# One reduction over 1152 columns instead of three partial ones: the row maximum of an attention score tile

## The chip, the cores and the metric

The program runs on one core of one Trainium2 chip. The metric is the device time of one execution in microseconds (us), of which the median of several runs is taken. A core has five engines that run their own instruction streams in order and meet at semaphores: TensorE (PE in the profile; its weight loads are PEld), VectorE (DVE), ScalarE (ACT), GpSimd (POOL) and SyncE (SP), which here issues the DMAs.

## The reference

Attention with queries pooled in pairs, then a soft mixture of experts, then a gated projection. The change is in the attention stage alone:

```python
def _attn_ref(q, k, v):          # 4 batches, 8 heads, 1152 positions, 64 wide
    q_pool = q.reshape(B, H, S // 2, 2, D).mean(axis=3)
    scores = scale * np.matmul(q_pool, k.transpose(0, 1, 3, 2))
    scores = scores - np.max(scores, axis=-1, keepdims=True)
    attn = np.exp(scores)
    attn = attn / (np.sum(attn, axis=-1, keepdims=True) + 1e-09)
    return np.matmul(attn, v)
...
x = moe(attn_out)                # 32 slots, 8 experts
g = x @ w_in - np.tanh(x @ w_in)
return g @ w_out
```

The kernel takes the row maximum over all 1152 keys before the exponential, as the reference does.

## The kernel before, in words

The attention stage goes over 16 pairs of heads. `over_pairs` writes out pairs 0, 1, 14 and 15 and puts pairs 2 to 13 into a loop of six passes with two pairs each; inside the loop the values that semaphores are waited for are computed in registers. A pair has twelve steps in a fixed order (`SEQ`): nine steps work on a tile of scores (T 0 to T 8: 128 queries by 1152 keys), and three prepare the next pair (Q at step 3, K at steps 6 and 9).

The scores of a tile lie in three banks of PSUM, 512, 512 and 128 columns (`CHUNK`), next to each other. Two such groups of banks ("slots") take turns, so the tile of step s reuses the slot of step s - 2. Around one tile the engines do this:

- TensorE in step s writes the three chunks of scores of step s's tile (`scores`, L304, two matmuls a chunk). Ahead of them it transposes chunks 0 and 1 of the probabilities of the tile of step s - 2 (`prob_chunk`, L320, eight transposes); this waits until the exponential of that tile is done (`exp_done`, L312). Between score chunks 1 and 2 it transposes the last block of that tile (L320, one transpose), which waits for VectorE's copy of chunk 1 (`second_evac`, L317). At the end of most steps come matmuls of transposed probabilities with V (`pv`, L337); steps 1, 3, 6 and 10 have none.
- VectorE in step s first copies chunk 1 of the transposed probabilities from PSUM to SBUF (L415, or L413 for the tile that mixes two heads; 512 columns). In steps 5 and 11 it then scales results (L447 to L461). After that it takes the partial maxima of score chunks 0 and 1, copies the last block of 128 transposed columns (`third`, L415), takes the partial maximum of chunk 2, and combines the three (L500) into one column of `neg_max`.
- ScalarE in step s copies chunk 0 of the transposed probabilities (L553) and then computes the exponential of the tile of step s - 1 over its 1152 columns (L542), which needs that tile's `neg_max` (`neg_done`). The exponential is followed by a read of its accumulator, the row sums.

Steps 5, 8 and 11 have no tile two steps back (a Q or K step lies there), so VectorE has no copies in them and TensorE no transposes of probabilities.

GpSimd prepares q and k of the next pair, SyncE loads k, q and v. Behind the attention stage follow the gating, the experts and the projection (`mlp`), which the change does not touch.

The tile step on VectorE is short enough to see here; L496 and L500 are the instructions that the change replaces:

Of the kernel before, what the change touches and what calls it, by code (L numbers as in the profile page):

```python
# [7 lines left out]
ALU = mybir.AluOpType  # L8
ACT = mybir.ActivationFunctionType
AX = mybir.AxisListType  # L10
P = 128
# [6 lines left out]
def attention(nc, dram, sizes, x, ident, rep, rep_ready, rep_step, early):  # L18
# [8 lines left out]
    CHUNK = [(0, 4), (4, 8), (8, 9)]  # L27
    NCH = len(CHUNK)
# [30 lines left out]
    with ExitStack() as ctx:  # L59
        def sb(name, shape, dt=F32):  # L60
            return ctx.enter_context(nc.sbuf_tensor(name, shape, dt))

        def sem(name):
            return ctx.enter_context(nc.semaphore(name))
# [15 lines left out]
        ones = sb("ones", [P, 1])  # L80
        ident_r = sb("ident_r", [P, P], F32R)
        outT = [sb(f"outT{g}", [P, GN[g]]) for g in range(2)]
        part_neg = sb("part_neg", [P, NCH])
        neg_max = sb("neg_max", [P, TILES])
        row_sum = [sb(f"row_sum{i}", [P, QT + 1, 2]) for i in range(2)]
        mix_sum = [sb(f"mix_sum{i}", [P, 1]) for i in range(2)]
# [6 lines left out]
        v_in = [sem("v_in0"), sem("v_in1")]  # L93
        zeroed, ident_ready = sem("zeroed"), sem("ident_ready")
        k_hi, k_split, q_sum = sem("k_hi"), sem("k_split"), sem("q_sum")
        part_done = sem("part_done")
        scores_full, neg_done, exp_done = sem("scores_full"), sem("neg_done"), sem("exp_done")
        ktr_full, k_evac, qtr_full, q_evac, q_high, q_low = (
            sem("ktr_full"), sem("k_evac"), sem("qtr_full"), sem("q_evac"), sem("q_high"), sem("q_low"))
# [11 lines left out]
        def wait(eng, s, value):  # L111

            if not isinstance(value, int) or value > 0:
                eng.wait_ge(s, value)
# [39 lines left out]
        def steps_of(last):  # L154
            return range(STEPS + DRAIN if last else STEPS)
# [83 lines left out]
        def slot_banks(s):  # L239
            return ps[:, 3 * (s % 2):3 * (s % 2) + 3, :]  # L240

        def slot_row(s):
            return slot_banks(s).rearrange("p b c -> p (b c)")[:, 0:S]
# [173 lines left out]
        def group_read(eng, p, j):  # L417

            if j == 0:
                wait(eng, pv_done, p * 2 - 1)  # L420
            elif j == G0:
                wait(eng, pv_done, p * 2)
# [8 lines left out]
        @block.vector  # L431
        def _(dve):
            dve.wait_ge(zeroed, 5)
            split(dve, 0)
            split_q(dve, 0, 0)

            def results(p, par, s, first):

                for g in range(2):
                    for b in (0, 1):  # L440
                        if OUT_STEP[g] == s + STEPS * b and not (b and first):
                            pp, q = p - b, par ^ b
                            if g == 0:

                                dve.wait_ge(exp_done, pp * TILES + TILES)
                                dve.wait_ge(mix_in, pp * 32 + 32)
                                nc.vector.tensor_scalar(row_den[:], row_sum[q][:], 1e-9, None, ALU.add).then_inc(den_done, 1)  # L447
                                dve.wait_ge(den_done, pp + 1)
                                nc.vector.reciprocal(row_inv[:], row_den[:]).then_inc(inv_done, 1)
                                dve.wait_ge(inv_done, pp + 1)  # L450
                            dve.wait_ge(otr_full, pp * 2 + g + 1)
                            n = 2
                            src = ps[:, TBANK, 0:n * P].rearrange("p (t h d) -> p t h d", t=n, h=2)
                            inv = row_inv[:, 2 * g:2 * g + n, :].unsqueeze(3).broadcast_to([P, n, 2, D])
                            dst = x[:, bass.ds(pp, 1), 2 * g:2 * g + n, :].rearrange("p o t (h d) -> p (o t) h d", h=2)
                            ins = nc.vector.tensor_tensor(dst, src, inv, ALU.mult)
                            if GN[g] > 2 * P:
                                src = ps[0:QR, TBANK, n * P:(n + 1) * P].rearrange("p (h d) -> p h d", h=2)
                                inv = row_inv[0:QR, QT, :].unsqueeze(2).broadcast_to([QR, 2, D])
                                dst = x[0:QR, bass.ds(pp, 1), QT, :].rearrange("p o (h d) -> p (o h) d", h=2)  # L460
                                ins = nc.vector.tensor_tensor(dst, src, inv, ALU.mult)  # L461
                            ins.then_inc(out_evac, 1)

            def body(p, par, first, last):
                for s in steps_of(last):
                    t2 = job_at(s, 2, first, last)
                    if t2 and t2[0] == "T":
                        _, j2, back = t2
                        pp = p - back
                        group_read(dve, pp, j2)  # L470
                        dve.wait_ge(ptr_full, (pp * TILES + j2) * NCH + 2)
                        evac_chunk(nc.vector.tensor_copy, s, j2, 1).then_inc(second_evac, 1)
                    results(p, par, s, first)

                    def third():

                        if t2 and t2[0] == "T":
                            dve.wait_ge(ptr_full, (pp * TILES + j2) * NCH + 3)
                            if job and job[0] == "T":
                                dve.wait_ge(scores_full, (p * TILES + job[1]) * NCH + 3)  # L480
                            elif job and job[0] == "K":
                                dve.wait_ge(ktr_full, (p + 1) * 2 + job[1] + 1)
                            elif job:
                                dve.wait_ge(qtr_full, p + 2)
                            evac_chunk(nc.vector.tensor_copy, s, j2, 2).then_inc(third_evac, 1)

                    job = job_at(s, 0, first, last)
                    if job and job[0] == "T":
                        tau = p * TILES + job[1]
                        j = job[1]  # L490
                        wait(dve, neg_done, tau)
                        for c in range(NCH):
                            if c == 2:
                                third()
                            dve.wait_ge(scores_full, tau * NCH + c + 1)
                            nc.vector.reduce_max(part_neg[:, c:c + 1], slot_banks(s)[:, c, 0:(CHUNK[c][1] - CHUNK[c][0]) * P], AX.X,  # L496
                                                 negate=True).then_inc(part_done, 1)
                        dve.wait_ge(part_done, tau * NCH + NCH)
                        wait(dve, exp_done, tau - TILES + 1)
                        nc.vector.tensor_scalar(neg_max[:, j:j + 1], part_neg[:, 0:1], part_neg[:, 1:2], part_neg[:, 2:3],  # L500
                                                ALU.min, ALU.min).then_inc(neg_done, 1)
                    else:
                        third()

            over_pairs(dve, body)

        @block.scalar
# [726 lines left out]
```

## Time and profile before

| | us |
|---|---|
| Median of 3 runs | 989.16 (988.77 to 993.28) |
| Profiled execution, its own time | 988.49 |
| Span of that execution in the trace | 986.7 |
| TensorE matmuls busy | 891.1 |
| VectorE busy | 597.8 |
| ScalarE busy | 497.0 |

The profile is of one execution. Its span leaves out 1.8 us that lie around the program. An engine's busy time is the sum over its instructions, over stages with different limits; where one engine waits for another is read from the idle time before an instruction and from what released it.

### The profile page before, as it was taken

To read this page: it belongs to the slowest core of one execution; us is meant where nothing else is said; L and a number is where in the kernel's file an instruction comes from. 1 tells how busy PE (TensorE), PEld (TensorE's weight loads), DVE (VectorE), ACT (ScalarE), POOL (GpSimd) and SP (SyncE) were. 2 spreads that over 40 slices of the span, in tenths; PEclk is the share of its full clock that TensorE was granted. 3 is DMA by queue.
4 is the path that set the end of the run, shared out by engine and by line. 5 is a ranking of instruction groups with operands and counts; after the bars stand their busy time and mean duration, and the time that the engine had idled before them with its cause. 6 is when DMAs were issued, how large, how long until landed. Compare 5 with 4: busy or idle time off the path is not lost. (4 is left out here: it accounts for less than half of the span.)

```text
span 986.7 us, 16399 instructions
## 1 busy us (share of the span) xinstructions
PE 891.1 (90%) x5707; PEld 644.4 (65%) x5707; DVE 597.8 (61%) x1175; ACT 497.0 (50%) x711; POOL 294.5 (30%) x207
## 2 busy tenths in 40 slices
PE   3999999999999999999999998876672899999998
PEld 2776776776776776776776765633231788888887
DVE  4676677677677677677677664420017866676770
ACT  1655555555555555555555553210016766666660
POOL 4353333333433333433433200000001343333441
PEclk9999999999999999999999999979885899999999
DMA  3312202202202202202202000949933100000000
GB/s 120 131 31 74 72 2 72 72 0 72 72 0 72 72 0 72 72 0 72 72 0 72 25 1 2 350 171 395 400 134 128 54 22 21 21 21 21 21 21 33
DMA packets 48865, 75.50 MB, mean 77 GB/s; under 512 B 5056, under 2 KB 23488, under 8 KB 48320
## 3 DMA queue, kind: packets, MB, share of 16 engines
q1 hardware_dynamic: 48832, 75.06, 22.3%
q8 instruction: 21, 0.34, 0.1%
q14 instruction: 12, 0.10, 0.0%
HBM read 70.32 MB, written 4.72 MB: 76 GB/s over the span
## 5 line engine op out<-in xcount | busy, mean ns | idle before, releaser
L496 DVE TENSOR_REDUCE part_neg<-ps 128x1 f32<-128x512 f32 (+1 forms) x432 | 220.8, 548 | 6.9 <-PE ps L304 6.6
L320 PE MATMUL ps<-ident,prob 128*128 128x128 f32 x1296 | 204.7, 285 | 19.1 <-DVE probT L415 9.2
L320 PEld LDWEIGHTS ps<-ident,prob 128*128 128x128 f32 x1296 | 143.2, 140 | 105.9 <-DVE probT L415 38.6
L415 DVE COPY probT<-ps 128x512 f32<-128x512 f32 (+1 forms) x256 | 125.1, 489 | 143.2 <-PE ps L320 116.8
L542 ACT ACTIVATE prob<-ps,neg_max 128x1152 f32<-128x1152 f32 x144 | 175.5, 1219 | 58.7 <-DVE neg_max L500 58.3
L304 PE MATMUL ps<-kT,qT_hi 128*128 128x512 f32 (+1 forms) x480 | 175.9, 383 | 5.3 <-DVE qT_lo L205 5.2
L553 ACT ACTIVATE probT<-ps 128x512 f32<-128x512 f32 x144 | 86.0, 597 | 171.6 <-PE ps L320 169.8
L337 PE MATMUL ps<-probT,v_nat 128*64 128x256 f32 (+1 forms) x1152 | 167.5, 417 | 0.5 <-DVE probT L415 0.5
L304 PE MATMUL ps<-kT,qT_lo 128*128 128x512 f32 (+1 forms) x480 | 159.3, 355 | 0.0
L1089 POOL TENSOR_TENSOR g_lo<-g,g_hi 128x1024 fp32r<-128x1024 f32 x36 | 86.5, 2404 | 134.7 <-ACT g_hi L1059 134.7
L1032 PE MATMUL ps<-w_hi,g_hi 128*128 128x512 f32 x288 | 113.9, 396 | 3.0 <-POOL g_lo L1089 3.0
L1032 PE MATMUL ps<-w_lo,g_hi 128*128 128x512 f32 x288 | 113.4, 394 | 0.0
L1032 PE MATMUL ps<-w_hi,g_lo 128*128 128x512 f32 x288 | 113.0, 392 | 0.0
L304 PEld LDWEIGHTS ps<-kT,qT_hi 128*128 128x128 f32 x480 | 95.2, 201 | 21.6 <-issue 11.2
L337 PEld LDWEIGHTS ps<-probT,v_nat 128*64 128x64 f32 x1152 | 72.1, 136 | 41.9 <-issue 0.8
L304 PEld LDWEIGHTS ps<-kT,qT_lo 128*128 128x128 f32 x480 | 90.4, 191 | 9.9
L189 POOL TENSOR_TENSOR q_dup<-q_nat 128x512 f32<-128x512 f32 x30 | 38.9, 1297 | 161.4 <-DMA q_nat_r<-in_q 161.4
L203 POOL TENSOR_TENSOR qT_hi<-q_raw,ones 128x1216 fp32r<-128x1216 f32 x15 | 33.2, 2214 | 178.3 <-PE ps L304 153.5
L1114 DVE SCALAR_TENSOR_TENSOR tv<-sq,ps 128x1024 f32<-128x1024 f32 x36 | 44.0, 1221 | 53.9 <-ACT ps L1068 53.9
L1066 ACT ACTIVATE sq<-ps 128x1024 f32<-128x1024 f32 x36 | 36.9, 1024 | 64.2 <-PE ps L1016 64.2
L1032 PEld LDWEIGHTS ps<-w_hi,g_hi 128*128 128x128 f32 x288 | 55.0, 191 | 14.1 <-POOL g_lo L1089 3.5
L1032 PEld LDWEIGHTS ps<-w_hi,g_lo 128*128 128x128 f32 x288 | 54.7, 190 | 11.7
(142 smaller groups left out, 1000.0 us busy)
## 6 DMA issues: line engine op xcount, KB each, us to landing
ring<-in_moe_w SPq DMA_DIRECT2D x10, 2048.0 KB, 20.1
k_nat<-in_k SPq DMA_DIRECT2D x16, 576.0 KB, 4.0
v_nat<-in_v SPq DMA_DIRECT2D x16, 576.0 KB, 5.2
q_nat<-in_q SPq DMA_DIRECT2D x32, 256.0 KB, 4.5
w_first<-in_moe_w SPq DMA_DIRECT2D x4, 2048.0 KB, 13.8
out<-res SPq DMA_DIRECT2D x18, 256.0 KB, 2.0
x<-in_moe_w SPq DMA_DIRECT2D x2, 2048.0 KB, 11.3
x<-in_moe_w_in SPq DMA_DIRECT2D x1, 4096.0 KB, 29.5
```

Source lines behind the costliest of these rows:

```text
L189: eng.tensor_tensor(q_dup[:, :, :, c, :], q_nat[:, :, :, 0, :], q_nat[:, :, :, 1, :], ALU.add).then_inc(q_sum, 1)
L304: last = nc.tensor.matmul(banks[:, c, 0:k1 - k0], stationary, kT[par][:, a, k0:k1], start=(n == 0), stop=(n == len(parts) - 1))
L320: last = nc.tensor.transpose(block_at(s, kt), src[:, kt * P:(kt + 1) * P], ident[:])
L337: last = nc.tensor.matmul(ps[64 * h:64 * h + D, VBANK, 0:n], v_nat[par][:, h, kt, :], probT[g][:, kt, h, :], start=(kt == 0), stop=(kt == ...
L415: return eng_copy(probT[g][:, k0:k1, h, col:col + P], src.rearrange("p (c q) -> p c q", c=n))
L496: nc.vector.reduce_max(part_neg[:, c:c + 1], slot_banks(s)[:, c, 0:(CHUNK[c][1] - CHUNK[c][0]) * P], AX.X, negate=True).then_inc(part_done, 1)
L542: nc.scalar.activation(prob[prob_index(par, n)][:], slot_row(s), ACT.Exp, bias=neg_max[:, n:n + 1], accum_out=sums).then_inc(exp_done, 1)
L553: evac_chunk(lambda d, s_: nc.scalar.activation(d, s_, ACT.Copy), s, j, 0).then_inc(first_evac, 1)
L1032: last = nc.tensor.matmul(ps[:, 2 * HB + i, :], a[par][:, ft, i * P:(i + 1) * P], w[:, ft, :], start=(ft == 0 and k == 0), stop=(ft == FT ...
L1066: nc.scalar.activation(sq[b % 2][:], h_of(b), ACT.Square, scale=(1.0 / 3.0) ** 0.5).then_inc(sq_done, 1)
L1089: nc.gpsimd.tensor_tensor(block_of(g_lo, par, b), g[b % 2][:], block_of(g_hi, par, b).bitcast(F32), ALU.subtract).then_inc(gl_done, 1)
L1114: nc.vector.scalar_tensor_tensor(tv[b % 2][:], sq[b % 2][:], 1.0, h_of(b), ALU.subtract, ALU.mult).then_inc(series_done, 1)
```

## The change

The three partial maxima with their semaphore `part_done`, the scratch tile `part_neg` and the combining instruction are gone. Instead the last block of transposed probabilities is copied first (`third`), and then one reduction reads all 1152 columns of the slot (`slot_row`, which ScalarE reads already) and writes the column of `neg_max` itself. It waits for the third chunk of scores; the waits for the first and the second, the wait for the previous tile's `neg_done` and the wait for `part_done` are gone too.

```diff
-        part_neg = sb("part_neg", [P, NCH])
...
-        part_done = sem("part_done")
...
-                        wait(dve, neg_done, tau)
-                        for c in range(NCH):
-                            if c == 2:
-                                third()
-                            dve.wait_ge(scores_full, tau * NCH + c + 1)
-                            nc.vector.reduce_max(part_neg[:, c:c + 1], slot_banks(s)[:, c, 0:(CHUNK[c][1] - CHUNK[c][0]) * P], AX.X,
-                                                 negate=True).then_inc(part_done, 1)
-                        dve.wait_ge(part_done, tau * NCH + NCH)
+                        third()
+                        dve.wait_ge(scores_full, tau * NCH + NCH)
                         wait(dve, exp_done, tau - TILES + 1)
-                        nc.vector.tensor_scalar(neg_max[:, j:j + 1], part_neg[:, 0:1], part_neg[:, 1:2], part_neg[:, 2:3],
-                                                ALU.min, ALU.min).then_inc(neg_done, 1)
+                        nc.vector.reduce_max(neg_max[:, j:j + 1], slot_row(s), AX.X, negate=True).then_inc(neg_done, 1)
```

## Rows read from the trace of the kernel before

**Rows 1.** The page: the span, then busy time, share and instructions of each engine.

```profile
span 986.7 us, 16399 instructions
PE 891.1 (90%) x5707; PEld 644.4 (65%) x5707; DVE 597.8 (61%) x1175; ACT 497.0 (50%) x711; POOL 294.5 (30%) x207
```

**Rows 2.** Busy time by windows, one pair of the loop: window, length, engines, granted clock, DMA.

```profile
199.96:236.81 36.85, 35.96 (x249) 25.82 (x247) 25.51 (x60) 20.58 (x33) 12.71 (x10) 1.00 0.16 48
```

**Rows 3.** Waits, 52 to 568 us: who waited for whom, total, times, longest.

```profile
ACT prob L542 <- DVE neg_max L500: 43.2, 29, 1.5
PEld ps L320 <- DVE probT L415: 30.5, 98, 0.4
PEld ps L320 <- ACT prob L542: 24.6, 64, 0.5
```

**Rows 4.** Groups by line and form, VectorE, 34 to 640 us: total, mean ns, idle before.

```profile
L496 DVE TENSOR_REDUCE part_neg<-ps 128x1 f32<-128x512 f32 x281 | 180.0, 681 | 5.3 <-PE ps L304 5.1
L415 DVE COPY probT<-ps 128x512 f32<-128x512 f32 x125 | 86.5, 692 | 113.3 <-PE ps L320 113.3
L496 DVE TENSOR_REDUCE part_neg<-ps 128x1 f32<-128x128 f32 x141 | 39.5, 280 | 0.0
L500 DVE TENSOR_SCALAR neg_max<-part_neg 128x1 f32<-128x1 f32 x141 | 38.6, 274 | 13.9
...
L758 DVE TENSOR_REDUCE col<-lT 128x1 f32<-128x576 f32 x1 | 0.8, 753 | 0.0
```

**Rows 5.** Timeline, VectorE, steps 1 and 2 of a loop pair: start, duration.

```profile
205.24 1.28 DVE L496 TENSOR_REDUCE part_neg<-ps 128x1 f32<-128x512 f32 x2
206.43 0.28 DVE L415 COPY probT<-ps 128x128 f32<-128x128 f32 x1
206.63 0.28 DVE L496 TENSOR_REDUCE part_neg<-ps 128x1 f32<-128x128 f32 x1
207.04 0.27 DVE L500 TENSOR_SCALAR neg_max<-part_neg 128x1 f32<-128x1 f32 x1
207.24 0.69 DVE L415 COPY probT<-ps 128x512 f32<-128x512 f32 x1
```

**Rows 6.** Timeline, TensorE and its weight loads, the same two steps.

```profile
205.37 0.14 PEld L320 LDWEIGHTS ps<-ident,prob 128*128 128x128 f32 x1 [0.29 <-DVE probT L415]
...
205.60 0.27 PE L304 MATMUL ps<-kT,qT_lo 128*128 128x128 f32 x1
206.04 1.09 PE L320 MATMUL ps<-ident,prob 128*128 128x128 f32 x8 [0.17 <-ACT prob L542]
...
207.99 0.14 PEld L320 LDWEIGHTS ps<-ident,prob 128*128 128x128 f32 x1 [0.36 <-DVE probT L415]
```

**Rows 7.** Timeline, ScalarE (step 11's end, step 2) and TensorE's first load of step 0.

```profile
199.50 0.19 ACT L542 ACTIVATION_READ_ACCUMULATOR prob<-ps,neg_max 128x1 f32 x1
199.96 0.85 PEld L320 LDWEIGHTS ps<-ident,prob 128*128 128x128 f32 x8 [0.49 <-ACT prob L542]
...
207.34 1.22 ACT L542 ACTIVATE prob<-ps,neg_max 128x1152 f32<-128x1152 f32 x1
```

**Rows 8.** Timeline, VectorE, step 8: three partial maxima with no copy between them.

```profile
226.11 1.49 DVE L496 TENSOR_REDUCE part_neg<-ps 128x1 f32<-128x512 f32 x3 [0.28 <-PE ps L304]
```

**Rows 9.** Timeline, TensorE and VectorE, the first pair (written out, not in the loop).

```profile
23.30 0.42 PE L304 MATMUL ps<-kT,qT_lo 128*128 128x128 f32 x1
24.36 0.27 DVE L500 TENSOR_SCALAR neg_max<-part_neg 128x1 f32<-128x1 f32 x1
26.03 1.09 PE L320 MATMUL ps<-ident,prob 128*128 128x128 f32 x8 [0.75 <-ACT prob L542]
...
29.17 0.28 DVE L496 TENSOR_REDUCE part_neg<-ps 128x1 f32<-128x128 f32 x1
29.48 0.27 DVE L500 TENSOR_SCALAR neg_max<-part_neg 128x1 f32<-128x1 f32 x1
...
36.28 1.09 PE L320 MATMUL ps<-ident,prob 128*128 128x128 f32 x8 [0.19 <-ACT prob L542]
```

## The prediction

> **What bounds the kernel now.** I read the page first. TensorE's matmuls are busy for 891.1 of 986.7 us, VectorE for 597.8 [rows 1]. The windows show the attention stage, the only one touched: a loop pair takes 36.85 us, of which TensorE is busy for 35.96 at the full granted clock (1.00, the 2.4 GHz level), VectorE for 25.51 and ScalarE for 20.58 [rows 2]. So the time saved on VectorE as such is worth nothing. What counts is the few tenths for which TensorE stands still in a pair, and whether the change makes them longer.
>
> The waits name them: TensorE's weight load at L320 waited 98 times for VectorE's copy (30.5 us) and 64 times for the exponential (24.6 us) [rows 3]. The exponential in turn waited 29 times for `neg_max` [rows 3]: the change acts through the time at which `neg_max` is there, and through the time at which VectorE is free for its next copy.
>
> **What VectorE's work costs before and after.** A partial maximum takes 681 ns over 512 columns and 280 over 128 [rows 4], so 401 ns for 384 columns: 1.044 ns a column on a fixed 146 ns. The one reduction of 576 columns in the kernel took 753 ns [rows 4] where this line gives 747. For 1152 columns it gives 146 + 1203 = 1349, say 1.35 us. Before, a tile costs 2 x 681 + 280 + 274 = 1.92 us of VectorE; after, 1.35. Over 144 tiles that is 0.57 x 144 = 82 us less VectorE work.
>
> The bounds of the 1.35: it is not in the trace of before. Below, ScalarE passes over the same 1152 columns in 1.22 us [rows 7], for another engine and operation. Above, three partial maxima in a row take 1.49 us for the same columns with three fixed costs [rows 8]. I take the line, since two sizes fix it and a third lies on it.
>
> **When the result is there.** This is step 1 of a loop pair, where VectorE is tightest. Before: partial maxima of chunks 0 and 1 from 205.24 on, the copy `third` at 206.43, the last partial maximum at 206.63, the combination from 207.04 to 207.31 [rows 5]. But TensorE had finished all scores at 205.60 + 0.27 = 205.87 [rows 6]. The first two maxima ran partly beside the scores, and this cover goes. After: the copy starts at 205.87 + 0.04 for the hand-over = 205.91; 0.04 is an estimate, since the partial maximum that waits for a matmul in step 8 starts directly behind it [rows 8] and TensorE starts 0.06 behind a copy (207.93 to 207.99) [rows 5, 6]. The reduction starts 0.20 after the copy, as 206.63 does after 206.43 [rows 5], at 206.11, and ends at 207.46. Before it was 207.31. So `neg_max` comes 0.15 us later, though VectorE works 0.57 us less. Removed are also the 0.13 us between the last partial maximum's end (206.91) and the combination (207.04) [rows 5]; they are in the 0.15.
>
> The waits in front: the reduction has two (scores, `exp_done`), where the partial maximum 0.20 behind its copy had one. In the loop a wait's value is computed first. One such wait behind `part_done` cost about 0.10: the combination starts 0.41 after the partial maximum in the loop (206.63 to 207.04) [rows 5], 0.31 in the pair written out (29.17 to 29.48) [rows 9]. Two are 0.20, just what the copy covers. I take 0, with up to 0.10 as the upper bound.
>
> **Where it lies on TensorE's path.** Going through the twelve steps:
>
> Step 1 into step 2. The next copy of 512 columns started at 207.24 with no idle time before it, because VectorE was still combining [rows 5]; TensorE's load behind it sat idle for 0.36 us, against 0.29 in the step before, where VectorE was free in time [rows 6]. This place is already VectorE's. After: the copy starts at 207.46 less the 0.07 by which the copy overlapped the combination = 207.39, 0.15 later, and TensorE's load and everything behind it shift by 0.15. Nothing gives it back: step 2 ends in V matmuls behind which step 3 starts at once. The exponential of step 1's tile, which began at 207.34 behind `neg_max` [rows 7], moves by the same 0.15 beside it. Cost: 0.15 in each of pairs 1 to 15, 2.3 us.
>
> Step 10 into step 0. Its exponential waits for `neg_max` too. Its accumulator read ended at 199.50 + 0.19 = 199.69, and TensorE started at 199.96 behind V matmuls [rows 7]. With the 0.06 of a hand-over 0.21 is spare, and 0.15 fits. This is the cover that goes next: of an extra x per tile, x - 0.06 is paid here as well.
>
> Steps 4 and 7. Their exponentials also start 0.15 later, but the tiles are transposed behind a step with V matmuls, with over half a microsecond to spare. Steps 0 and 2: the exponential waits for ScalarE's copy, not for `neg_max`. Steps 5, 8 and 11 have no copies: here the old partial maxima ended at 226.11 + 1.49 = 227.60 plus a combination [rows 8], and one reduction behind the last score ends within 0.3 us of that on either side; VectorE's next copy there waits for TensorE. Cost 0. The copy `third` comes about 0.5 us earlier everywhere; who waits for it (`pv`, the K and Q copies) waits for something later. No DMA moves.
>
> Pair 0 has no V matmuls as cover. Its first tile: scores end at 23.30 + 0.42 = 23.72, the combination at 24.63 [rows 9]. After: 23.72 + 0.04 + 1.35 = 25.11, 0.48 later; its two big partial maxima had run beside the scores. TensorE already waits 0.75 for this exponential at 26.03 [rows 9], so all of it is paid. At two more places of this pair, the starts of steps 4 and 6 (36.28, where TensorE waits 0.19 for the exponential [rows 9]), the shift is paid as 0.15 + 0.10, for here the combination had followed without the 0.10. Together 0.48 + 0.5 = 1.0 us.
>
> **Sum.** 2.3 + 1.0 = 3.3 us. On the profiled execution 988.49 + 3.3 = 991.8. The median of the runs is 0.67 above that execution, so 989.16 + 3.3 = 992.5 us, 0.33% slower. By the bounds, x from -0.13 (reduction 1.22) to +0.24 (1.49, and 0.10 for the waits): an extra x costs 18x, for 15 pairs and three places of pair 0, and from 0.06 on 15(x - 0.06) at step 0. That is 3.3 - 2.3 = 1.0 to 3.3 + 4.3 + 2.7 = 10.3 us, or 990.2 to 999.5.
>
> **A rule against this sum.** VectorE is busy 25.51 of 36.85 us of a pair [rows 2], and only one of its twelve copies of chunk 1 starts without idle time before it for want of VectorE. The Trainium skill (VectorE: DVE Perf Modes, Rules for kernel authors) advises for chained VectorE operations to minimize the number of operations, since each pays its pipeline flush. By that the four instructions made one would gain: it is rival B below. The rule counts VectorE's work and leaves out that the first two instructions ran beside the matmuls.
>
> **Rivals.**
>
> A, slower by over 0.5%. The reduction over three banks costs more than the line, or the waits in front of it are not covered. Each tile's `neg_max` is then x later again, and step 0 starts to be late in each pair besides step 2. Against the limit of 4.9 us (about 0.5%, what a measurement of this kernel can tell from no change): 3.3 + 18x + 15(x - 0.06) = 4.9 at x = 0.08, a reduction of 1.43 us. With x = 0.13: 3.3 + 2.3 + 1.1 = 6.7, so 995.9. For it: little is needed, and 1.49 is a row. Against: the line fits three sizes, and the kernel's other engine reads across the banks without trouble. 0.25.
>
> B, faster. VectorE's relief wins where it was late. The place is step 2's copy alone; it can win back the 0.07 by which that load waits longer than others (0.36 to 0.29 [rows 6]): 15 x 0.07 = 1.1 us, to 988.1. It decides at a reduction of 1.20 us, under the lower bound. For it: 82 us less VectorE work. Against: nearly all VectorE idle time before copies is waiting for TensorE's transposes (113.3 us [rows 4]). Faster by over 0.5% would need a wait that I have not found. 0.09, and 0.04 beyond 0.5%.
>
> C, nothing to see. The later `neg_max` is absorbed everywhere but in pair 0, because step 2's late load is made up for behind it: 989.16 + 1.0 = 990.2. For it: 0.15 us is small. Against: step 2 ends in matmuls that start as soon as the load is through. 0.12.
>
> **How the numbers follow.** My forecast has 0.50, A 0.25, C 0.12, B 0.13 in all. Within 0.5%: 0.50 + 0.12 + 0.09 = 0.71; slower 0.25; faster 0.04. The range reaches down to C and B's near side, 989.0, and up into A as far as the upper row (6.7 us and a little scatter), 996.5.
>
> **What would show it.** The reduction at 1.35 us; in a loop pair the copy in step 2 starting 1.35 instead of 1.20 us behind the first transpose, and the load behind it idle for 0.5; a loop pair of 37.00 instead of 36.85; VectorE's busy time down by about 80 us, TensorE's the same; step 0 started by V matmuls, not by the exponential. The prediction is wrong if pairs shorten, or if step 0 or a step other than 2 starts later against its predecessor.

## The result, and the profile after

The changed kernel takes 997.3 us in the median of 18 runs (989.88 to 999.81), the kernel before 990.15 in the median of 18 (986.16 to 994.76): a ratio of 1.0061 with a 95% interval of 1.0042 to 1.0080. It is slower, by about 6 us by the ratio; the two medians stand 7.15 apart. The forecast was 0.33% slower, 992.5 us with a range to 996.5. By the ratio, 0.61% is 995.2 on the scale of the forecast, inside the range; the median of 997.3 as it stands is 0.8 above its end. Either way the result lies on the side beyond 0.5% that had a chance of 0.25.

The profiled execution took 995.59 us. Its page, span and busy times:

```profile
span 993.8 us, 15680 instructions
PE 896.6 (90%) x5707; PEld 647.1 (65%) x5707; DVE 546.0 (55%) x743; ACT 498.0 (50%) x711; POOL 294.6 (30%) x207
```

VectorE is busy for 52 us less while the kernel takes longer, and TensorE's matmuls take 5.5 us more [rows 1]. The groups of the same stretch on VectorE, by line and form (L492 is the one reduction, L413 the copies that were L415; TensorE's transposes of probabilities, L320 before, are L318 now):

```profile
L492 DVE TENSOR_REDUCE neg_max<-ps 128x1 f32<-128x1152 f32 x141 | 190.2, 1350 | 19.3 <-PE ps L302 19.1 <-issue 0.2
L413 DVE COPY probT<-ps 128x512 f32<-128x512 f32 x125 | 86.3, 691 | 109.4 <-PE ps L318 109.4
L413 DVE COPY probT<-ps 128x128 f32<-128x128 f32 x126 | 36.8, 292 | 74.5 <-PE ps L302 47.0 <-PE ps L279 15.7 <-PE ps L287 9.7
```

The reduction takes 1350 ns, as the line through 280 and 681 [rows 4] said (these rows count 141 tiles, since the window leaves out the first ones). The copy of the last block, 128 columns, now has idle time before it (47 us of it until the scores are complete): that idle time is the lost cover, since before VectorE spent it on the first two partial maxima.

Steps 1 and 2 of a loop pair, VectorE, to be laid beside [rows 5]:

```profile
207.81 0.29 DVE L413 COPY probT<-ps 128x128 f32<-128x128 f32 x1 [0.59 <-PE ps L302]
208.02 1.35 DVE L492 TENSOR_REDUCE neg_max<-ps 128x1 f32<-128x1152 f32 x1
209.28 0.68 DVE L413 COPY probT<-ps 128x512 f32<-128x512 f32 x1
```

And TensorE's weight loads of the same steps, beside [rows 6]:

```profile
207.27 0.14 PEld L318 LDWEIGHTS ps<-ident,prob 128*128 128x128 f32 x1 [0.29 <-DVE probT L413]
...
207.94 0.86 PEld L318 LDWEIGHTS ps<-ident,prob 128*128 128x128 f32 x8 [0.31 <-ACT prob L533]
...
210.02 0.14 PEld L318 LDWEIGHTS ps<-ident,prob 128*128 128x128 f32 x1 [0.49 <-DVE probT L413]
```

The copy of step 2 starts 1.34 us behind its transposes (207.94 to 209.28), where it was 1.20, and TensorE's load waits 0.49 us instead of 0.36. The windows of two consecutive loop pairs, beside [rows 2], each from the start of a step 0 to the next:

```profile
164.83:201.85 37.02, 36.07 (x248) 25.89 (x247) 22.26 (x33) 20.60 (x33) 13.88 (x11) 1.00 0.16 48
201.85:238.86 37.01, 36.09 (x248) 25.81 (x246) 22.42 (x33) 20.60 (x33) 12.51 (x10) 1.00 0.17 48
```

(The first window begins 0.1 us early: step 0 starts at 164.93, so that pair takes 36.92.) From the start of TensorE's first transposes of the gating, 617.91 us before and 621.21 now, the attention stage is 3.30 us longer, of which 0.06 lie ahead of its first matmul: 3.24 us are the change's. The other 3.8 us of the 7.1 by which the span grew arise behind it, where both programs have the same instructions.

Where in a pair the time went, worked out from the starts of TensorE's loads in both traces. Even pairs are the first, odd pairs the second of the two in a pass of the loop. The first three columns are the length of a part of the pair in us; steps 10 and 11 are those just ahead of this pair's step 0, and the fourth column is the pair with them; the windows above run from step 0 to step 0 and put this stretch into the pair before, so the longer one there (37.01) is an odd pair and here (37.03) an even one. The last is how far behind its transposes the last block's load of step 2 starts:

| loop pair | step 9 | steps 10 and 11 ahead | step 2 | pair | load in step 2 |
|---|---|---|---|---|---|
| before, even / odd | 2.95 / 2.95 | 5.43 / 5.45 | 3.43 / 3.40 | 36.86 / 36.84 | 1.95 |
| changed, even / odd | 2.88 / 2.88 | 5.56 / 5.42 | 3.55 / 3.52 | 37.03 / 36.90 | 2.08 |

All other steps are the same to 0.02. So step 2 costs 0.12 to 0.13, the start of step 0 comes 0.11 to 0.13 later in the even pairs and not in the odd ones, and step 9 gives 0.07 back. In the pairs that are written out, step 2 costs 0.20 (pairs 1, 14 and 15), step 9 gives nothing back, and step 0 of pairs 14 and 15 is on time; into pair 2, the first of the loop, step 0 costs 0.20. In pair 0 the shifts of TensorE's starts are 0.48, 0.31 and 0.32 at steps 2, 4 and 6 (against 26.03, 31.16 and 36.28 before), 1.1 us.

### The profile page after: what moved, and what is told of

Read it like the earlier page. It is cut to its first block and busy times, and to the rows that moved or that the text cites. A ratio compares the mean times of both kernels' runs of the same rounds, so it can differ in the third digit from the quotient of the medians.

```text
span 993.8 us, 15680 instructions
## 1 busy us (share of the span) xinstructions
PE 896.6 (90%) x5707; PEld 647.1 (65%) x5707; DVE 546.0 (55%) x743; ACT 498.0 (50%) x711; POOL 294.6 (30%) x207
## 5 line engine op out<-in xcount | busy, mean ns | idle before, releaser
L413 DVE COPY probT<-ps 128x512 f32<-128x512 f32 (+1 forms) x256 | 125.8, 491 | 186.7 <-PE ps L318 112.8
L318 PE MATMUL ps<-ident,prob 128*128 128x128 f32 x1296 | 204.7, 285 | 20.3 <-ACT prob L533 8.9
L318 PEld LDWEIGHTS ps<-ident,prob 128*128 128x128 f32 x1296 | 143.3, 140 | 108.6 <-DVE probT L413 40.1
L492 DVE TENSOR_REDUCE neg_max<-ps 128x1 f32<-128x1152 f32 x144 | 194.3, 1350 | 22.6 <-PE ps L302 22.4
L1105 DVE SCALAR_TENSOR_TENSOR tv<-sq,ps 128x1024 f32<-128x1024 f32 x36 | 44.0, 1222 | 54.2 <-ACT ps L1059 54.2
```

Of the source, the lines that this page charges most:

```text
L318: last = nc.tensor.transpose(block_at(s, kt), src[:, kt * P:(kt + 1) * P], ident[:])
L413: return eng_copy(probT[g][:, k0:k1, h, col:col + P], src.rearrange("p (c q) -> p c q", c=n))
L492: nc.vector.reduce_max(neg_max[:, j:j + 1], slot_row(s), AX.X, negate=True).then_inc(neg_done, 1)
L1105: nc.vector.scalar_tensor_tensor(tv[b % 2][:], sq[b % 2][:], 1.0, h_of(b), ALU.subtract, ALU.mult).then_inc(series_done, 1)
```

## The experiments

All kernels ran beside the kernel before on the same chips. "Gating at" is the start of the gating stage in the profiled execution, 617.91 before, so its difference is what the attention stage lost or won, but for 0.0 to 0.3 us by which the first matmuls of each execution come earlier or later (5.65 in later_start, by intent). The part behind is the span less this start, 368.8 before and 372.6 in the changed kernel.

| kernel | gating at | even / odd loop pair | load in step 2 | part behind | median us (runs) | ratio and interval |
|---|---|---|---|---|---|---|
| one_tile_single | 620.74 | 36.98 / 36.96 | 2.08 | 369.2 | 992.79 (12) | 1.0020 (1.0000 to 1.0040) |
| other_tiles_single | 620.62 | 36.90 / 36.75 | 1.95 / 1.93 | 370.7 | 992.98 (12) | 1.0024 (1.0003 to 1.0044) |
| parts_late | 639.04 | 38.12 / 37.93 | 2.63 | 374.7 | 1014.05 (4) | 1.0219 (1.0178 to 1.0261) |
| two_parts | 623.22 | 37.27 / 37.06 | 2.19 | 370.4 | 995.44 (12) | 1.0045 (1.0027 to 1.0063) |
| changed_again | 621.06 | 37.03 / 36.89 | 2.08 | 370.1 | 994.78 (12) | 1.0045 (1.0026 to 1.0064) |
| late_start | 617.85 | 36.86 / 36.82 | 1.95 | 369.4 | 990.94 (12) | 1.0015 (0.9999 to 1.0032) |
| first_then_rest | 617.56 | 36.81 / 36.77 | 1.97 / 1.95 | 373.0 | 991.18 (12) | 1.0005 (0.9987 to 1.0023) |
| fewer_columns | 616.59 | 36.71 / 36.68 | 1.87 | 370.1 | 988.65 (10) | 0.9989 (0.9973 to 1.0005) |
| later_start | 624.20 | 36.85 / 36.83 | 1.95 | 368.1 | 994.61 (8) | 1.0037 (1.0018 to 1.0056) |
| fill_in_step_1 | 619.52 | 36.91 / 36.94 | 2.01 / 2.05 | 371.1 | 991.71 (10) | 1.0018 (0.9993 to 1.0043) |

### one_tile_single and other_tiles_single: the change for one tile of nine, and for the other eight

`alone(j)` is `j == 1` in the first, `j != 1` in the second; the other branch is the kernel before's.

```diff
+                        if alone(j):
+                            third()
+                            dve.wait_ge(scores_full, tau * NCH + NCH)
+                            wait(dve, exp_done, tau - TILES + 1)
+                            nc.vector.reduce_max(neg_max[:, j:j + 1], slot_row(s), AX.X, negate=True).then_inc(neg_done, 1)
+                        else:
...
```

> The kernel before, with the one reduction only for the tile of step 1 of each pair; the other eight tiles keep three partial maxima. Theory (the copy of step 2 is the place): the copy in step 2 starts 1.35 instead of 1.20 us behind its transposes, 15 pairs x 0.15 = 2.3 us plus 0.25 in pair 0, so the attention stage ends about 2.5 us later than in the kernel before (617.9 to 620.4). Step 0 and step 9 stay as they were. Rival (the cost is spread over all tiles, because reading three banks in one instruction is slow or disturbs the others): a ninth of 3.3, 0.4 us.

> The complement: the one reduction for all tiles but that of step 1. Theory: nothing at step 2 (its copy starts at 1.20 again); pair 0 costs 0.5 for its first tile and 0.25 for step 6; step 0 costs 0.17 in every second pair as in the changed kernel (1.2 us), the shorter hand-over at step 9 gives 0.07 back in each pair (1.0 us): attention stage 0.5 to 1.0 us later than before. Rival (spread cost): eight ninths of 3.3, 2.9 us.

With the single reduction in step 1 alone the load of step 2 is at 2.08 and the loop pair takes 0.12 us longer; nothing else in it moves. One tile of nine makes 2.7 us (620.74 less 617.91, less 0.16 for its start), of which 2.0 lie in pairs 1 to 15 and 0.7 in pair 0, where 0.25 was expected. A ninth of 3.24 would be 0.36. The cost has a place, and the spread-cost rival is out.

The other eight tiles leave step 2 at 1.95. In their loop pairs they cost 0.11 to 0.13 at step 0 of every second pair, and win 0.07 at step 9 of each: on average 36.83 against 36.85 before, nothing. Their gating still starts at 620.62, 2.45 us late beyond the start; I had expected 0.5 to 1.0. The difference is in pair 0. TensorE's matmuls over 512 columns in this kernel:

```profile
29.39 0.63 PE L309 MATMUL ps<-kT,qT_hi 128*128 128x512 f32 x1
29.82 0.56 PE L309 MATMUL ps<-kT,qT_lo 128*128 128x512 f32 x1
```

Here they took 0.63 us until 29.8 us into the span. In the kernel before the same kind went over to 0.40 at 24.5, in the changed kernel by 27.7:

```profile
24.05 0.59 PE L304 MATMUL ps<-kT,qT_lo 128*128 128x512 f32 x1
24.48 0.40 PE L304 MATMUL ps<-kT,qT_hi 128*128 128x512 f32 x1
```

The trace's record of the granted clock begins just there: at 24.5 us in the kernel before, at 26.0 in the changed kernel, at 30.2 here. For the time ahead of its first record a window shows 1.00 for want of one, which says nothing of the clock. Ahead of it two such matmuls start 0.43 us apart (22.34 and 22.77 in the kernel before), behind it 0.23 (24.48 and 24.71), close to the ratio of the two levels, 1.2 and 2.4 GHz; that the first microseconds ran at the lower level is read from this, not from a recorded grant. The two intervals from step 2 to step 4 of pair 0 are 1.83 us longer here than before and 0.31 longer in the changed kernel, so the late speeding-up is worth about 1.5 of the 2.45 us. What is left, 0.9 to 1.0, is the expectation's upper end. Whether the eight tiles have a part in the late speeding-up one execution can't show.

### parts_late: the order without the fusion

Three partial maxima and the combination as before, but all behind the copy `third` and behind the last score.

```diff
                         wait(dve, neg_done, tau)
+                        third()
+                        dve.wait_ge(scores_full, tau * NCH + NCH)
                         for c in range(NCH):
-                            if c == 2:
-                                third()
```

> Three partial maxima and their combination, but behind the copy of the last block and behind all scores, as the one reduction is. This isolates the lost cover from the saved instructions. Theory: the maximum is there 1.49 + 0.13 + 0.27 us behind the copy instead of 1.35, 0.54 later than with the one reduction and 0.7 later than before. 15 x 0.7 at step 2, 15 x 0.5 or more at step 0, some 2.5 in pair 0: attention stage 18 to 24 us later than in the kernel before. Rival (order and cover do not matter, only the work of VectorE counts): the same as before, within 1 us.

The attention stage is 21 us longer. The load of step 2, in the timeline of TensorE's weight loads, waits 1.03 us where the changed kernel's waits 0.49:

```profile
216.92 0.14 PEld L320 LDWEIGHTS ps<-ident,prob 128*128 128x128 f32 x1 [1.03 <-DVE probT L415]
```

This separates the two halves of the change. To take the first two maxima out from beside the matmuls costs 21 us; to make one instruction of four gives 18 of them back. The change is the small difference of two large effects: a tile's 0.15 of the forecast is the 0.7 that the expectation above gives for the lost cover, less about 0.55 for the saved instructions.

### two_parts: fused, but ahead of the copy

```diff
-                        for c in range(NCH):
...
+                        dve.wait_ge(scores_full, tau * NCH + 2)
+                        nc.vector.reduce_max(part_neg[:, 0:1], slot_row(s)[:, 0:8 * P], AX.X, negate=True).then_inc(part_done, 1)
+                        third()
```

> Cover kept, one instruction fewer: one reduction over the 1024 columns of score chunks 0 and 1 ahead of the copy, one over the last 128, and a combination of two. Theory: VectorE is through 0.05 to 0.07 us earlier than before at step 2, which is all that can be won there; 15 x 0.06 = 0.9, and with what step 9 won in the changed kernel up to 2 us earlier: attention stage 0.5 to 2 us shorter, total not to be told from before. Rival (fewer instructions as such do it): as the changed kernel or faster than before by over 3 us.

The expectation was wrong. The attention stage is 5.3 us longer, where the changed kernel's is 3.2 longer. VectorE in steps 1 and 2:

```profile
207.78 1.23 DVE L493 TENSOR_REDUCE part_neg<-ps 128x1 f32<-128x1024 f32 x1 [0.23 <-PE ps L304]
208.92 0.28 DVE L415 COPY probT<-ps 128x128 f32<-128x128 f32 x1
209.12 0.28 DVE L496 TENSOR_REDUCE part_neg<-ps 128x1 f32<-128x128 f32 x1
209.52 0.21 DVE L499 TENSOR_SCALAR neg_max<-part_neg 128x1 f32<-128x1 f32 x1
209.70 0.69 DVE L415 COPY probT<-ps 128x512 f32<-128x512 f32 x1
```

The reduction over 1024 columns is 0.05 us shorter than the two over 512, but it stands idle 0.23 us for the scores of chunk 1, for which the first of the two never waited. With the combination still behind it VectorE is through later than with one reduction over everything. I had counted the instruction saved and overlooked the cover lost in it, which is the error that this change invites. In the trace the combination of step 1 ends at 209.73, 4.01 us behind the transposes of the step (205.72), against 3.82 before and 3.98 in the changed kernel.

### first_then_rest: fused where nothing is covered

```diff
+                        dve.wait_ge(scores_full, tau * NCH + 1)
+                        nc.vector.reduce_max(part_neg[:, 0:1], slot_row(s)[:, 0:4 * P], AX.X, negate=True).then_inc(part_done, 1)
+                        third()
+                        dve.wait_ge(scores_full, tau * NCH + 3)
+                        nc.vector.reduce_max(part_neg[:, 1:2], slot_row(s)[:, 4 * P:9 * P], AX.X, negate=True).then_inc(part_done, 1)
```

> Two reductions: chunk 0 (512 columns) before the copy of the last block, as soon as its scores are there, then chunks 1 and 2 in one over 640 columns, and a combination of two. Cover kept, one instruction fewer. Theory: the copy ends 0.6 us earlier than in the kernel before but has to wait for all scores, so it starts 0.04 behind them as in the changed kernel; the second reduction takes 146 + 668 = 0.81 us, the combination 0.13 + 0.21: the maximum is there at 205.91 + 0.20 + 0.81 + 0.34 = 207.26 on the scale of the kernel before, against 207.31. Step 2's load 0.05 earlier, step 9 perhaps 0.07, no cost at step 0; pair 0 within 0.2. Attention stage 0.5 to 2 us shorter than before, total not to be told from it. Rival (fused reductions cost more than separate ones whatever their place, as two_parts seems to say): 3 to 5 us longer.

The timeline of VectorE, step 1 and the first copy of step 2:

```profile
205.43 0.68 DVE L493 TENSOR_REDUCE part_neg<-ps 128x1 f32<-128x512 f32 x1
206.11 0.29 DVE L415 COPY probT<-ps 128x128 f32<-128x128 f32 x1
206.31 0.81 DVE L496 TENSOR_REDUCE part_neg<-ps 128x1 f32<-128x640 f32 x1
207.25 0.21 DVE L499 TENSOR_SCALAR neg_max<-part_neg 128x1 f32<-128x1 f32 x1
207.45 0.69 DVE L415 COPY probT<-ps 128x512 f32<-128x512 f32 x1
```

The 640 columns took 0.81 us, as the line says. Loop pairs are 0.05 to 0.07 us shorter than before, all of it at step 9; step 2 is not earlier (1.97 and 1.95), where 0.05 had been expected. The gating starts 0.35 us earlier, less than the 0.5 to 2 expected. The total, 1.0005 (0.9987 to 1.0023), is not to be told from the kernel before: the fused form that keeps the cover costs nothing, and here it won nothing that the total shows. Its part behind the attention, 373.0 us, is as long as the changed kernel's 372.6, so a long one does not need the changed kernel.

### fewer_columns: a cheaper reduction in the changed order

The maximum leaves out the last 192 of the 1152 columns.

```diff
-                        nc.vector.reduce_max(neg_max[:, j:j + 1], slot_row(s), AX.X, negate=True).then_inc(neg_done, 1)
+                        nc.vector.reduce_max(neg_max[:, j:j + 1], slot_row(s)[:, 0:7 * P + 64], AX.X, negate=True).then_inc(neg_done, 1)
```

> The changed kernel with its one reduction over 960 of the 1152 columns; the last 192 are left out of the maximum. By the line of 146 ns and 1.044 a column it takes 1.15 us instead of 1.35. Theory (place and size of the reduction set the cost): step 2's copy is no longer late (load 1.88 to 1.95 behind its transposes instead of 2.08), step 0 starts as before, pair 0 costs 0.4; attention stage between 1.7 us shorter and 0.4 longer than in the kernel before. Rival (the changed order costs as such): still 2 us or more longer.

The group of the reduction on VectorE, 34 to 640 us:

```profile
L492 DVE TENSOR_REDUCE neg_max<-ps 128x1 f32<-128x960 f32 x141 | 162.0, 1150 | 22.6 <-PE ps L302 22.5 <-issue 0.2
```

1150 ns, 0.20 less, and everything that the change costs in a loop pair is gone: step 2's load at 1.87, its step 0.06 to 0.07 shorter than in the kernel before, step 0 on time, 36.7 a pair. Pair 0, without cover, still costs 0.5 us. The gating starts 1.3 us earlier than before. So in the loop the order as such costs nothing; the length of the uncovered piece decides, and the point where it turns lies between 1.15 and 1.35 us; the forecast had put it at 1.20.

### fill_in_step_1: the suspected lateness alone

The kernel before with a fill of a scratch tile of 128 columns behind the combination in step 1.

```diff
                                                 ALU.min, ALU.min).then_inc(neg_done, 1)
+                        if j == 1:
+                            nc.vector.memset(blank[:], 0.0)
```

> The kernel before with one fill of 128 columns on VectorE behind the combination of step 1 in each pair, 0.1 to 0.17 us of VectorE's time ahead of the copy of step 2; all else untouched. Theory (it is the lateness of that copy that costs, not what makes it late): the load of step 2 at 2.05 to 2.1 behind its transposes instead of 1.95, the pair 0.1 to 0.17 longer, attention stage 1.6 to 2.6 us longer; step 9 and step 0 as in the kernel before. Rival (the copy is released by TensorE alone and VectorE's lateness is hidden): no change, within 0.3 us.

The timeline of VectorE at the end of step 1 and the start of step 2:

```profile
207.63 0.27 DVE L501 TENSOR_SCALAR neg_max<-part_neg 128x1 f32<-128x1 f32 x1
207.88 0.17 DVE L504 MEMSET blank<- 128x128 f32 x1
207.96 0.68 DVE L416 COPY probT<-ps 128x512 f32<-128x512 f32 x1
```

Work of 0.17 us, most of which the next copy overlaps, still makes each loop pair 0.05 to 0.10 us longer (one of the twelve 0.34) and the attention stage 1.6; the load of step 2 sits at 2.01 and 2.05. VectorE's lateness at this one place reaches TensorE whatever makes it late. Step 9 and step 0 are as before.

### changed_again, late_start and later_start: the part behind the attention

> The changed kernel as it is, once more, beside the three others. The attention stage accounted for 3.2 us of its loss; the profile lost 3.8 more behind it, where no instruction differs. Theory (the stages behind end earlier or later by how long TensorE's granted clock stays at its lower level, in every execution anew): attention stage again 3.2 to 3.4 us longer, the part behind it anywhere between 368 and 375 us, median 993 to 997. Rival (the longer tail belongs to this kernel): part behind again 372 or more in the profile and a median again 6 to 7 us above the kernel before.

The second profile of the changed kernel has the same attention stage (3.15 us longer) and a part behind of 370.1 instead of 372.6. Its median is 4.7 us above the kernel before beside it, so neither the long tail of the first profile nor its 7 us come again in full.

```diff
+            for n in range(3):
+                wait(dve, blanked, n)
+                nc.vector.memset(blank[:], 0.0).then_inc(blanked, 1)
             split_q(dve, 0, 0)
```

> The kernel before with three fills of a scratch tile on VectorE (3.3 to 3.6 us in all) ahead of the first q preparation, so that everything behind them starts later and nothing else changes. Theory: pairs take 36.85 us as before, the gating starts 3.3 to 3.6 us later than 617.9, the total is 3.5 us longer with the same scatter as before. Rival (the stages behind the attention take longer because they start later against something fixed in the chip): total 6 to 7 us longer, as in the changed kernel, whose gating starts at the same time.

This experiment did not do what it was for: VectorE waits 6.2 us for q at that place in the kernel before, the fills ran in that time (11.49 to 15.35) and delayed nothing. It stands as a repeat of the kernel before. later_start puts the three fills (950 columns each) inside `split_q`, behind its waits.

```diff
             wait(eng, scores_full, (n - 1) * TILES * NCH)
+            if isinstance(n, int) and n == 0:
+                for m in range(3):
+                    wait(eng, blanked, m)
+                    eng.memset(blank[:], 0.0).then_inc(blanked, 1)
```

> As late_start, but the three fills (about 1.15 us apart) stand behind the wait for q, where VectorE is needed at once, so that the first scores come 3.2 to 3.5 us later and the pairs are left as they are. Theory (the part behind the attention varies by its clock, whatever stands before): pairs 36.85, gating at 621.2 as in the changed kernel, total 3.3 us above the kernel before at equal granted clock (993 where the mean is 0.967, 995.6 where it is 0.962 to 0.964). Rival (a start of the gating at about 621 us is what makes the part behind longer and the low clock more frequent): median 996 to 998, two executions in three or more at 0.964 or lower.

First scores at 27.00 instead of 21.35, more than planned because the first product behind the fills took 3.29 us (1.43 in the kernel before), and the gating at 624.20, 3 us later than in the changed kernel. Yet the part behind was 368.1 us, the shortest of all, and only one of eight runs had a mean granted clock under 0.966. A late start of the gating did not make what follows longer. The gating of one_tile_single and other_tiles_single starts within 0.6 us of the changed kernel's, and 18 of their 24 runs had 0.966 or more.

What does vary is TensorE's clock. One window of 20 us over the same work of the gating in each profile, starting 23.0 us behind its first transposes, first the kernel before, then the changed one (window, length, busy PE, PEld, DVE, ACT, POOL, granted clock, DMA share, GB/s):

```profile
640.91:660.91 20.00, 12.28 (x81) 5.34 (x85) 7.24 (x14) 4.13 (x6) 1.80 (x1) 0.79 0.33 117
```

```profile
644.21:664.21 20.00, 15.08 (x73) 6.70 (x73) 7.27 (x14) 3.89 (x6) 0.00 (x0) 0.59 0.29 107
```

A mean of 0.59 is four fifths of the window at the 1.2 GHz level (0.50), 0.79 two fifths. In both traces the grant fell in a stretch in which TensorE mostly waited for the small steps of the softmax between its matmuls (in the kernel before it was busy for 0.35 of the 1.5 us from 639.0 on and for 0.49 of the next 1.5; the grant fell at about 642), but in the changed kernel it fell 1.7 us earlier in this work (643.9 against 642.3, the gating having started 3.3 later), stayed down for 10 us where it had been 7, came back at about 654, and fell again at 657. The stretch's matmuls over c_parts took 3.20 us before and 5.23 now, the 40 over d_nat 6.78 and 7.61, and the experts start 2.9 us later beyond the 3.3. Over all of the part behind, the clock records give 63.0 us at the lower level in the kernel before, 75.4 in the changed kernel and 69.9 in its second profile. Of the twelve profiles the three with the longest part behind (372.6, 373.0 and 374.7) have 75.1 to 76.8 us of it, the three with the shortest (368.1, 368.8 and 369.2) 63.0 to 63.2. By the mean granted clock of each run:

| | runs at 0.966 or more | their median | runs below | their median |
|---|---|---|---|---|
| kernel before (three series) | 51 | 989.5 | 32 | 992.3 |
| changed kernel (both series) | 9 | 992.2 | 21 | 997.5 |

Among runs at the higher mean clock the change costs 2.7 us, close to what the attention stage shows. The rest of the 6 us comes from the other half of the table: the changed kernel was more often in it (21 of 30 against 32 of 83), and lost more there. The excess is in its first series, 15 of 18, for which the clock of the kernel before beside it is not on record; in the second it was 6 of 12 against 14 of 35 beside it.

## Why the prediction was right in its sum, and where it was not

**The price of the reduction, 1.35 us**: measured 1350 ns; 1024 columns 1222 ns, 960 columns 1150 ns, 640 columns 0.81 us. The line through two sizes held at four more.

**82 us less VectorE work**: the durations of VectorE's instructions, summed over the trace, fell by 83.0 us (648.4 to 565.4), but its busy time by 52. Neighbouring instructions overlap at their ends, the busy time counts such a stretch once, and the four short ones of before overlapped more. The forecast's sign "busy time down by about 80 us" took the one for the other, and that of TensorE's unchanged busy time failed too (5.5 more). The forecast also speaks of twelve copies of chunk 1 in a pair; there are nine, of which one starts without idle time before it. Its sum uses none of these.

**When the maximum is there, 0.15 later**: copy at the scores' end, reduction 0.20 or 0.21 behind it, no extra for two waits in the loop. Measured against the transposes of the step, step 1's reduction ends at 209.37 - 205.39 = 3.98 instead of 207.31 - 203.49 = 3.82: 0.16.

**Step 2's copy, 0.15 in 15 pairs**: in the loop pairs 0.12 to 0.13, in the pairs written out 0.20; there the combination had followed without the 0.10 for the wait's value, which the forecast counted in pair 0 alone. Shown three ways: by the one tile alone, by its absence in the other eight, by a mere fill in the same place.

**Step 0, spare 0.21, so no cost**: this step of the forecast failed, and by its own sign ("if step 0 ... starts later") the forecast was wrong here. Into the even pairs TensorE came 0.11 to 0.13 us later. The exponential's accumulator read ended at 238.44 + 0.19 = 238.63, and TensorE's load followed only at 238.86. The timelines of ScalarE and of TensorE's loads, and the view of line 112, where the kernel's `wait` asks for a semaphore, between 238 and 239 us (PEldq is the sequencer in front of the loads; it gives durations in ns, then the first and last start in us):

```profile
238.44 0.19 ACT L533 ACTIVATION_READ_ACCUMULATOR prob<-ps,neg_max 128x1 f32 x1
```

```profile
L112 PEldq ALU_OP  x1: 36/36/36, 238.7 to 238.7; - x1
L112 PEldq FUSED_REGOPS  x1: 51/51/51, 238.8 to 238.8; - x1
```

```profile
238.86 0.75 PEld L318 LDWEIGHTS ps<-ident,prob 128*128 128x128 f32 x7 [0.60 <-issue]
```

A hand-over of 0.23, not the 0.06 that I took from another place. Between the end of the exponential and the load stand two register instructions, 0.10 apart, in which the values of the waits behind the first (`first_evac`, `out_evac`) are computed; so the late exponential is waited for first and the rest of the list is worked off after it. This is so only at the step 0 with which a pass of the loop begins. Everywhere else that TensorE waited for an exponential, in both traces, its load followed 0.05 us behind the accumulator read, in steps 2 and 7 too, which have the same third wait by the code; into the odd pairs it followed 0.10 us behind it and on time. With 0.23 the spare was 0.04. The forecast read its 0.21 at 199.96 [rows 7], the start of an odd pair, where it held. That the register instructions make the 0.23 is read from their place in the trace; no run changed them alone.

**Step 9, not in the forecast**: 0.07 won in each loop pair. The load of step 9 was 1.95 behind its transposes before, as in step 2, and 1.88 now. It is not VectorE's being late, for its copy there had been waiting for over a microsecond. The copy itself started 1.20 behind the transposes before and 1.13 now. First the kernel before (load, VectorE's wait for the transposes from the view of line 471, copy), then the changed one (load, copy):

```profile
228.40 0.85 PEld L320 LDWEIGHTS ps<-ident,prob 128*128 128x128 f32 x8 [0.49 <-issue]
L471 DVEq EVENT_SEMAPHORE  x1: 21/21/21, 229.5 to 229.5; - x1
229.60 0.69 DVE L415 COPY probT<-ps 128x512 f32<-128x512 f32 x1 [1.60 <-PE ps L320]
```

```profile
230.42 0.85 PEld L318 LDWEIGHTS ps<-ident,prob 128*128 128x128 f32 x8 [0.49 <-issue]
231.55 0.69 DVE L413 COPY probT<-ps 128x512 f32<-128x512 f32 x1 [1.34 <-PE ps L318]
```

Step 9 has two waits ahead of its copy, for V matmuls long done (`pv_done`) and for the transposes. In the kernel before the one for the transposes is an instruction of its own, which runs when they are done, and the copy follows it by 0.06; in the changed kernel it sits on the copy. The traces of one_tile_single, two_parts and fill_in_step_1, which won nothing there, show the separate instruction in all twelve loop pairs; those of other_tiles_single, parts_late, first_then_rest and fewer_columns, which won, in none. Pairs 1, 14 and 15, written out, have it in the changed kernel too, and won nothing. So the 0.07 come from how the two waits were laid out in the loop, not from the reduction; what decides the layout was not looked into.

**Pair 0, 1.0 us**: measured 1.1, in the three places named.

**The sum, 3.3 us**: the attention stage lost 3.24. By its parts: step 2 2.2 (12 loop pairs at 0.12 to 0.14, three others at 0.20), pair 0 1.1, step 0 0.8 (0.20 into pair 2, 0.11 to 0.13 into five others), step 9 minus 0.8 (12 pairs). That it met to a tenth is partly luck: the last two, neither in the forecast, cancel.

**Behind the attention, nothing**: this is what the forecast of the total lacked. Among the twelve profiles the part behind was 368.1 to 374.7 us, with the same instructions in all. Rival A, slower by over 0.5%, came out in size, but not by its mechanism: the reduction cost what the line says and the waits before it nothing. Its late step 0 came, in every second loop pair, for the reason above. Rival B's case, that fewer operations win, is refuted: two_parts, with one operation fewer, lost 5.3 us. Where an instruction stands outweighs how many there are, for parts_late, with as many as before, lost 21. But the saved instructions are worth much, 18 us against parts_late. The Trainium skill's advice to minimize the number of operations (VectorE: DVE Perf Modes, Rules for kernel authors) holds in this trace with the order held the same, by those 18 us, and not against the kernel before, by 3.2; it does not say what the operations ran beside. Rival C, absorbed lateness, is out.

Left open: whether the changed kernel falls to the lower clock more often by what it is, or whether 18 runs of its first series happened to. Only the start time of the gating was excluded as the cause. So about half of the 6 us is shown, the other half is a share of the clock whose cause is open, and that the total fell into the forecast's range owes something to both.

## What to carry to other kernels

Before fusing partial reductions that run behind the pieces of a matmul, find when the last input is there and count from then on: what stands behind it after the change (here 0.20 + 1.35 us) against what stood behind it before (1.40, the first pieces being done). Fewer instructions and 52 us less of VectorE's busy time lost 3 us, because the first two of the instructions had been free. If one fuses at all, fuse only the pieces whose inputs come last: 512, then 640, cost nothing.

A spare time at a hand-over has to be read at that very place, and in every kind of pass: the 0.06 of one wait was 0.23 at the top of the loop, and the kernel lost 0.8 us by it, while the pair from which the spare had been read lost nothing. Where several waits stand ahead of an instruction in a loop, it counts which of them comes last in the list: what is behind the late one is worked off after it, here 0.18 us at one place and 0.07 at another.

## What the runs showed that was not expected

The same stages behind the attention took 368.1 to 374.7 us in twelve profiles, with runs at a mean granted clock from 0.960 to 0.972, and the medians of the kernel before differed by 2.8 us between the two halves of that range. An effect of 3 us in one stage has to be read from that stage; totals need the granted clock beside each run, and even 30 and 83 runs did not settle it.

At the start of the program TensorE's matmuls over 512 columns took 0.63 us for the first 3 to 9 us of the score matmuls, ahead of the first record of the granted clock in each trace; how long differed from execution to execution and was worth about 1.5 us once.
